# A rewritten first stage and an output stored by tile, in an mLSTM attention kernel with two dense layers

## The reference, cut to what is computed

```python
for t in range(S):
    m_new = np.maximum(f_gate[:, :, t] + m, i_gate[:, :, t])
    f_stab = np.exp(f_gate[:, :, t] + m - m_new)
    i_stab = np.exp(i_gate[:, :, t] - m_new)
    m = m_new
    C = f_stab * C + i_stab * outer(v_t, k_t)
    n = f_stab * n + i_stab * k_t
    y[:, :, t] = sigmoid(o_gate) * (C @ q_t) / maximum(abs(n @ q_t), 1.0)
h = x @ w_in                                   # 320 -> 2048
x = (maximum(h, 0) + alpha * minimum(h, 0)) @ w_out
out = maximum(maximum(x @ w1, x @ w2), x @ w3) @ w_out2   # 320 -> 768 -> 320
```

## Time and profile before

| | us |
|---|---|
| median of 3 runs | 790.53 (790.06 to 791.54) |
| the profiled execution | 790.44 |
| its span, first to last instruction | 788.7 |
| busy TensorE, VectorE, ScalarE, GpSimd | 742.5, 478.6, 309.9, 184.6 |

### The profile page before, as it was taken

How to read it: one execution, slowest core, us unless ns; L and a number is a source line. 1 busy time by engine, 2 the same in 40 slices (tenths; PEclk the granted TensorE clock), 3 DMA queues, 4 the chain that set the end, 5 groups by cost and what they waited for, 6 DMA issues and landing times.

```text
span 788.7 us, 11547 instructions
## 1 busy us (share of the span) xinstructions
PE 742.5 (94%) x4410; PEld 655.7 (83%) x4410; DVE 478.6 (61%) x823; ACT 309.9 (39%) x648; POOL 184.6 (23%) x187
## 2 busy tenths in 40 slices
PE   2556999999999999999999999999999999999997
PEld 2546999999998888888888888888888888888886
DVE  6456888878978786888688754934242332434222
ACT  4443465465456444644554245431111212121211
POOL 4376433335524332434233200000000000000000
PEclk9767999999999999999999999999999999999999
DMA  6961332222223221231110053030010202000000
GB/s 204 288 198 52 93 97 84 81 82 99 74 88 97 99 66 65 80 105 61 41 54 0 1 180 125 1 105 9 29 47 0 74 1 74 0 34 1 34 0 34
DMA packets 40057, 56.37 MB, mean 71 GB/s; under 512 B 3457, under 2 KB 29058, under 8 KB 39618
## 3 DMA queue, kind: packets, MB, share of 16 engines
q1 hardware_dynamic: 39570, 54.57, 22.0%
q10 hardware_dynamic: 432, 1.06, 0.4%
HBM read 47.65 MB, written 7.96 MB: 71 GB/s over the span
## 4 chain that ended last, share of the span: by engine, by line
PE 83%; DVE 7%; DMA 3%; POOL 3%; issue 1%; ACT 1%; SPq 1%; ACTq 0%; DVEq 0%; POOLq 0%
PE bank L664 25%; PE bank L628 20%; PE bank L642 5%; PE bank L643 5%; PE bank L644 5%; PE bank L554 4%; PE bank L678 3%; PE bank L679 3%; PE bank L680 3%; PE bank L646 3%; PE bank L647 3%; PE bank L562 1%; PE bank L569 1%; POOL wproj L369 1%; PE bank L591 1%
## 5 line engine op out<-in xcount | busy, mean ns | idle before, releaser
L628 PE MATMUL bank<-x_split,w_hi 128*128 128x512 f32 (+2 forms) x560 | 170.6, 372 | 2.2 <-ACT x_split L760 2.2
L628 PE MATMUL bank<-x_split,w_lo 128*128 128x512 f32 (+2 forms) x336 | 122.0, 365 | 0.0
L628 PEld LDWEIGHTS bank<-x_split,w_hi 128*128 128x128 f32 x560 | 103.8, 191 | 15.9 <-ACT x_split L760 2.6
L796 ACT ACTIVATE g_full<-bank 128x512 f32<-128x512 f32 (+2 forms) x112 | 59.7, 533 | 143.4 <-PE bank L628 141.7
L994 DVE SCALAR_TENSOR_TENSOR g_full<-g_full,beta,bank 128x512 f32<-128x512 f32 (+2 forms) x112 | 74.6, 667 | 38.2 <-ACT g_full L796 37.4
L642 PE MATMUL bank<-g_hi,wproj 128*128 128x512 f32 (+2 forms) x224 | 84.8, 379 | 4.0 <-DVE g_lo L975 4.0
L805 ACT ACTIVATE g_hi<-g_full 128x512 fp32r<-128x512 f32 (+2 forms) x112 | 63.1, 564 | 62.3 <-DVE g_full L994 62.1
L1015 DVE TENSOR_TENSOR best<-bank,first_of_max 128x512 f32<-128x512 f32 x36 | 24.9, 692 | 102.8 <-PE bank L664 76.4
L644 PE MATMUL bank<-g_hi,wproj 128*128 128x512 f32 (+2 forms) x224 | 81.3, 363 | 0.0
L643 PE MATMUL bank<-g_lo,wproj 128*128 128x512 f32 (+2 forms) x224 | 81.3, 363 | 0.0
L975 DVE TENSOR_TENSOR g_lo<-g_full,g_hi 128x512 fp32r<-128x512 f32 (+2 forms) x112 | 70.1, 626 | 18.1 <-ACT g_hi L805 17.3
(11 more groups left out here) (115 smaller groups left out, 1400.2 us busy)
## 6 DMA issues: line engine op xcount, KB each, us to landing
u_bcast<-u_scratch SPq DMA_DIRECT2D x24, 512.0 KB, 4.3
kv<-in_kv SPq DMA_DIRECT2D x24, 324.0 KB, 3.2
out<-final SPq DMA_DIRECT2D x6, 640.0 KB, 3.8
q_t<-in_q_t SPq DMA_DIRECT2D x24, 120.0 KB
k_t<-in_k_t SPq DMA_DIRECT2D x48, 60.0 KB
wproj_raw<-in_w_out SPq DMA_DIRECT2D x4, 640.0 KB, 9.6
o_gate<-in_o_gate SPq DMA_DIRECT2D x4, 640.0 KB, 5.0
w_raw<-in_w_max SPq DMA_DIRECT2D x2, 1152.0 KB, 6.5
```

The costliest lines, as they stand in the source:

```text
L628: ins = pe.matmul(ps[:, 0:cols], w[:, a, f], xs[:, x, 0:cols], start=(m == 0), stop=(m == 7))
L796: act.activation(gf[:, n % GF_SLOTS, 0:cols], hid[j % HID_BANKS][:, 0:cols], ACT.Relu, scale=-1.0).then_inc(neg_done, 1)
```

## The change

- **TensorE** starts with 20 products of zeros (`STILL`).
- **Gates** are worked out in two spans, chunks 0 and 1 of each batch, then chunks 2 to 5 (`SPANS`), in steps `chain`, `exps`, `turns` and `tables` that stand in the plan among the others.
- **u** of chunks 0 and 1 does not go through memory: TensorE spreads it by products with one-hot rows (`pick`) on top of a product that puts the mask there (`later`), and ScalarE reads it from PSUM. From chunk 2 on it is as before; ScalarE issues the store and the first load itself.
- **The decays** of the state come from a product with a one-hot row (`last`), in step `decays`, behind the first hidden tile of block 0; the state of chunk 1 is made after that (`late`). Chunk 0 needs no carry.
- **Weights** come in quarters, in the order in which block 0 uses them (`pieces`), all loaded by SP. All 16 low pieces are GpSimd's, each cut into operations of 256 columns (2 for one of w_in, 5 for one of w_out); the last eight lie around and inside block 0.
- **Loads**: chunk 1, the input gate and the first output gate are issued by ScalarE. Clearing of k moves from GpSimd to VectorE.
- **The end**: TensorE signals each of the last four tiles, ScalarE and VectorE copy two each, and each has its own store.

```diff
+ON_PE = PLAIN
+STILL = 20
+SPANS = [(0, ON_PE), (ON_PE, CPS)]
...
-    steps = [("prepare", 0), ("prepare", 1), ("gate", 0, 0), ("gate", 0, 1), ("scores", 0), ("carry", 0),
-             ("gate", 1, 0), ("gate", 1, 1), ("values", 0), ("scores", 1), ("finish", 0, 0), ("finish", 0, 1),
-             ("prepare", 2), ("carry", 1), ("values", 1), ("gate", 2, 0), ("gate", 2, 1), ("pack", 2, 0),
-             ("finish", 1, 0), ("finish", 1, 1), ("pack", 2, 1), ("prepare", 3)]
-    return steps + [("turn", 0), ("turn", 1)]
+    return [("chain", 0), ("exps", 0), ("turns", 0), ("bcast", 0), ("products", 0), ("tables", 0), ("gate", 0, 0),
+            ("gate", 0, 1), ("turns", 1), ("chain", 1), ("bcast", 1), ("scores", 0), ("tables", 1), ("prepare", 0),
+            ("chain", 2), ("values", 0), ("carry", 0), ("gate", 1, 0), ("gate", 1, 1), ("exps", 1), ("prepare", 1),
+            ("products", 1), ("scores", 1), ("finish", 0, 0), ("finish", 0, 1), ("carry", 1), ("values", 1),
+            ("turn", 0), ("turns", 2), ("finish", 1, 0), ("finish", 1, 1), ("tables", 2), ("turn", 1),
+            ("prepare", 2), ("gate", 2, 0), ("gate", 2, 1), ("pack", 2, 0), ("pack", 2, 1), ("prepare", 3)]
...
+        if b == 0 and n == 0:
+            both += [("decays",), ("late", 1)]
...
-PIECES = [("in", a, half) for half in range(2) for a in range(3)] + [("out", n, 0) for n in range(4)]
-ACT_PIECES = {("gate", 0, 1): (2, 3), ("gate", 1, 1): (3, 5), ("gate", 2, 1): (5, 6), ("pack", 2, 1): (6, 10)}
-DVE_PIECES = {("carry", 0): (2, 3)}
-POOL_PIECES = {("prepare", 2): (3, 5), ("prepare", 3): (5, 10)}
+    return [p for q in range(IN_PARTS) for p in [("in", a, q) for a in range(3)] + [("out", q, 0)]]
+ACT_PIECES = {("gate", 0, 1): (0, 3), ("exps", 1): (3, 7), ("turn", 0): (7, 8), ("gate", 2, 1): (8, 11),
+              ("hidden", 0, 1): (11, 12), ("hidden", 0, 2): (12, 15), ("hidden", 0, 3): (15, 16)}
+POOL_PIECES = {("prepare", 0): (0, 4), ("prepare", 1): (4, 8), ("pack", 2, 1): (8, 11), ("scores", 2): (11, 12),
+               ("carry", 2): (12, 15), ("carry", 3): (15, 16)}
+LOAD_U_AFTER = ("exps", 1)
...
+            sp.wait_ge(q_cleared, 1)
+            sp.wait_ge(k_cleared, 1)
+            load_chunk(sp, 0)
+            load_w1(sp, 0, range(3))
+            load_out(0)
+            load_w1(sp, 1, range(3))
+            sp.wait_ge(k_cleared, 3)
+            load_chunk(sp, 2)
+            load_out(1)
+            load_w1(sp, 2, range(3))
+            load_out(2)
+            load_w1(sp, 3, range(3))
+            load_out(3)
+            load_chunk(sp, 3)
+            sp.wait_ge(gates_done, 2)
+            for b in range(1, B):
+                store_u(sp, 0, b, u_stored[1])
+            sp.wait_ge(u_stored[0], 16)
+            load_u(sp, 3)
...
+            for n in range(STILL):
+                pe.matmul(ring[2][:, :], still[:, 0:128], still[:, :], start=True, stop=True)
...
+            def bcast(ch):
...
+                    for k in range(HG):
+                        pe.matmul(ps[:, k * L:(k + 1) * L], ident_b[:, :], later[:, :], start=(k == 0), stop=False,
+                                  skip_group_check=True)
+                    for k in range(HG):
+                        ins = pe.matmul(ps[:, k * L:(k + 1) * L], pick[:, g * HG + k, :], gates[:, U, t],
+                                        start=False, stop=True, skip_group_check=True)
...
             for s in PLAN_FIRST:
                 attention(s)
+                if s == LOAD_U_AFTER:
+                    act.wait_ge(u_stored[0], 16)
+                    load_u(act, ON_PE)
...
+            def last_tile(t):
+                act.wait_ge(tile2_out, t + 1)
+                act.activation(final[:, (NBLK2 - 1) % 2, t, :], acc2[t][:, 0:DM], ACT.Copy).then_inc(tile_ready[t], 1)
```

More of the change, by code:

```diff
@@ L222, in build @@
         end_at = cursor[0]
+        pick, _ = sb("pick_head", [128, H, L], F32, prob_r_at)
+        last, _ = sb("last_row", [128, 128], F32, prob_3_at)
+        later, _ = sb("later_keys", [128, 128], BF16, prob_3_at + 512)
+        ident_b, _ = sb("ident_bf16", [128, 128], BF16, prob_3_at + 768)
+        still, _ = sb("still", [128, 512], BF16, prob_at)
         cursor[0] = att_at
@@ L526, in drained, with decays @@
+            def decays():
+                pe.wait_ge(last_set, 1)
+                pe.wait_ge(tables_set, 3)
+                pe.matmul(acc[0][:, 256:256 + NCH * H], last[:, :], tables[:, 1, :, :].rearrange("p c h -> p (c h)"),
+                          start=True, stop=True).then_inc(decays_out, 1)
             def drained(n):
@@ L556, in attention @@
                         ins.then_inc(scored, 1)
-                if kind == "carry":
+                if kind == "carry" and ch:
                     ps = task("carry", ch)
@@ L564, in attention @@
                     ins.then_inc(carry_out, 1)
+                if (kind == "carry" and ch != 1) or kind == "late":
                     ps = task("state", ch)
@@ L673, in project2 @@
                 pe.wait_ge(g2_ready, b2 * J2 + f + 1)
+                last = b2 + 1 == NBLK2 and f + 1 == J2
                 for t in range(TT2):
@@ L720, in sigmoid, with exps @@
                 act.activation(og[:, b % 2, 0:n, :], og[:, b % 2, 0:n, :], ACT.Sigmoid).then_inc(o_done, 1)
-            sigmoid(0)
-            for half in range(2):
-                act.wait_ge(gates_done, half + 1)
-                if not half:
-                    ins = act.activation(gates[0:B * H, E, L:HALF], gates[0:B * H, U, L:HALF], ACT.Exp)
-                else:
-                    ins = act.activation(gates[0:B * H, E, HALF:S], gates[0:B * H, U, HALF:S], ACT.Exp)
-                for c in range(half * CPH, (half + 1) * CPH):
+            def exps(p):
+                first, end = SPANS[p]
+                act.wait_ge(gates_done, p + 1)
+                if p:
+                    store_u(act, ON_PE, 0, u_stored[0])
+                t = slice(max(first, 1) * L, end * L)
+                act.activation(gates[0:B * H, E, t], gates[0:B * H, U, t], ACT.Exp)
+                for c in range(first, end):
                     t = slice(c * L, (c + 1) * L)
@@ L733, in _ @@
                 ins.then_inc(exps_done, 1)
-                if not half:
-                    for n in range(2):
-                        high_piece(n)
+            sigmoid(0)
             def attention(step):
-                kind, ch = step[0], step[1]
+                kind = step[0]
+                if kind == "decays":
+                    return
+                ch = step[1]
                 c = ch % SLOTS
@@ L849, in _ @@
                 high2(b2, J2 - 1)
[L850 removed]
+                if b2 + 1 < NBLK2:
+                    final2(b2)
+            act.wait_ge(out_stored[(NBLK2 - 1) % 2], 16 * ((NBLK2 - 1) // 2))
+            for t in range(0, TT2, 2):
+                last_tile(t)
         @block.vector
@@ L895, in attention @@
             def attention(step):
-                kind, ch = step[0], step[1]
-                if kind in ("prepare", "gate", "pack", "sigmoid"):
+                kind = step[0]
+                if kind in ("prepare", "gate", "pack", "sigmoid", "exps", "turns", "bcast", "products"):
                     return
+                if kind == "decays":
+                    return set_decays()
+                ch = step[1]
+                if kind == "chain":
+                    return chain(ch)
+                if kind == "tables":
+                    return set_tables(ch)
                 c = ch % SLOTS
@@ L923, in attention @@
                                       .to_broadcast([128, NK, KH, DE]), ALU.mult).then_inc(carried_in, 1)
+                if (kind == "carry" and ch != 1) or kind == "late":
+                    if ch == 0:
+                        dve.wait_ge(own_set, 1)
                     ps = ring[TASKS.index(("state", ch)) % RING_BANKS]
```

402 lines of the change are left out of this document (240 added, 162 removed).

## The result

| | before | after |
|---|---|---|
| median, us | 791.03 (790.06 to 791.88, 4 runs) | 786.45 (785.84 to 787.38, 4 runs) |
| the profiled execution | 790.44 | 787.06 |
| its span | 788.7 | 785.1 |

The ratio is 0.9939, 95% interval 0.9923 to 0.9955: 4.6 us faster, where 9.5 were forecast. The profiled pair shows 3.4, because its run of before lies 0.6 under that median and its run of after 0.6 above. Single runs of one kernel differ by 1 to 2 us either way, so sums made from one profile can't be held to less than that.

The account below looks back on a forecast made before the run. TensorE was taken to set the pace from about 75 us on, so the front's shift counts: 790.44 - 9.7 (front) + 2.5 (back in block 0) - 2.2 (end) = 781.0 us, range 773.5 to 787.5.

Parts of the forecast that it names:

- What bounds the kernel: From about 75 us to the end only TensorE's own work sets the pace; a first-stage change shifts block 0's start.
- Gates and ScalarE up to the exponentials: First stage: first signal of the gates at 8.8, ScalarE's first gates from 11.6, exponentials of four chunks done at 20.5.
- The store of u: On ScalarE's own queue: leaves at 18.3, takes about 2.2 us, hidden up to 20.5.
- Rival (c): ScalarE's wait on u's store replaces the removed wait: at 7.23 us the chain starts 4.7 later, 785.7; chance 0.15.
- masks that wait for a DMA of u: Sign that the forecast is wrong: GpSimd's masks wait for this instead of for its own pieces.
- GpSimd as the chain of the front: GpSimd's 16 low pieces set the front: third state at 59.6 instead of 69.29, 9.7 us earlier.
- The zeros: 20 TensorE matmuls at the start speed chunk 0's broadcast: taken as 0, bounds a loss of 1.2 and a gain of 1.5.
- What comes back in block 0: GpSimd's pieces 12 to 15 inside block 0 contend with VectorE: 2.5 us back, bounds 0 and 7.9.
- The end: Last tiles' copies hidden behind TensorE, then a DMA of 160 KB: 2.2 us saved, 1.0 to 2.7.
- (b): GpSimd's quarter operations cost 0.59 instead of 0.72 and nothing comes back in block 0: 774.7; chance 0.2.
- (d): GpSimd and VectorE hold each other up in every small operation, 1.19 us each: 793.6, slower than before; chance 0.07.
- (e): u or weights land so late that block 0 starts where it did: 788.2, or 790.7 with 2.5 back; chance 0.03.

Follow-up runs that it names:

- the run with the weights held: SP holds the third quarter of w_in until u is stored, against the kernel with pieces put into the waits: 777.39 us, ratio 0.9833.
- the same kernel without the hold: After with low pieces 4 to 7 on VectorE, 8 to 10 moved ahead and 15 behind the pack of chunk 4: 777.47 us.
- with the wait moved: After with ScalarE's wait for the store of u and the load of u put behind high pieces 3 to 6: 782.21 us, ratio 0.9887.
- Filling the hole: After with 26 products of 256 columns added on TensorE ahead of the wait of project step 7 of block 0, for timing alone: 784.64 us.
- without any piece: After with the last four low pieces cut to 8 columns each, TensorE multiplying high parts in their place: 783.45 us, ratio 0.9910.
- piece 15 later: After with GpSimd's low piece 15 moved from behind the decay of chunk 3 to behind the last pack step of chunk 4: 785.58 us.
- VectorE's pieces: After with low pieces 4 to 7 moved from GpSimd to VectorE: 781.77 us; together with ScalarE's wait behind high pieces 3 to 6: 783.25 us.

## Why the prediction was half right

- **What bounds the kernel**: right. From rows to TensorE's last product nothing changed, 674.6 us in both.
- **Gates and ScalarE up to the exponentials**: right within 0.5 us (first products on gates at 8.96, forecast 8.8; first gate at 11.89, forecast 11.6; exponentials done at 21.0, forecast 20.5).
- **The store of u**: the step that failed. I gave it about 2.2 us of latency, hidden up to 20.5, because it has a queue to itself. It took from 18.88 to about 24.6, 5.7 us, and ScalarE stood still for 4.03. Rival (c) had this mechanism, at 4.7 later; the row of 7.23 us was there and should have been taken. That (c)'s 785.7 lies so near to 786.45 is in part luck: its wait is 0.7 too long (and counts the 0.4 for issuing the load on one side only), its block 0 gives back 2.4 too little. The sign that I gave for it, masks that wait for a DMA of u, did not show either; the wait sat on ScalarE, one step earlier. The store's own queue did not spare it the wait: DMA share in 20:30 was 1.09. The Trainium skill (DMA: Bandwidth & Descriptors, Queues, rings and completion order) says that each DMA engine takes its packets from the rows with work in turn. The trace agrees as far as the run with the weights held goes: 4.2 us from the issue of the store to that of the load behind it, against 5.9 in the same kernel without the hold. No run shows whether such turns make up the rest of the wait.
- **GpSimd as the chain of the front**: right in mechanism and size. From the late piece on my walk is off by 0.6 us in 36.6; a 256-column operation took 0.69 to 0.78 there, and with the wait moved the third state fell on 59.39.
- **The zeros**: taken as 0, measured at 2.1. The step said that ScalarE's list covers the broadcast until 11.6. At the slow rate it covers only the first half of it (ScalarE waits 1.10 us for the second), and not the scores behind it on TensorE, for which VectorE waits with the next gate chain behind it. My upper bound was 1.5. This adds nothing to the miss, since the forecast was for the kernel with the zeros.
- **What comes back in block 0**: 2.5 forecast, 4.9 measured, inside the bounds of 0 and 7.9. I had priced contention for VectorE's two-input operations and left out what follows. This is the second step that failed. One term was missing: VectorE operations that stand ahead of g_lo and are held up open a hole on TensorE (3.25 us), and behind it the clock is at half. Filling the hole gave 2.7 us of distance and 1.8 of the median. The last paragraph of my prediction named the clock as a sign but had no term for it.
- **The end**: right, 2.15 in the trace and 2.0 alone. Nothing between the last copy at 782.61 and the span's end at 785.1 but the issue and landing of 160 KB: 2.5 us, as taken.
- **Rivals (b), (d) and (e)**: GpSimd's 256-column operations cost neither 0.59 nor 1.19 but 0.69 to 0.78 on the chain, and 0.80 to 0.87 beside a busy VectorE. None of the three happened.

With the measured terms the sum closes, as it must, since they are all read from the two traces: 790.44 - 6.3 + 4.9 - 2.15 + 0.2 (1.96 us around the span instead of 1.74) = 787.1, the profiled run of after. Left open: the 1.8 to 2.0 us of distance that stay without any piece, and with piece 15 later (41.4 and 41.6 against 39.6). TensorE is idle 3.7 us on this way in both, against 1.7 before, so it is all idle time: without any piece nearly all in waits for g_lo, with piece 15 later 2.8 for g_lo and 0.8 for GpSimd's split. Part is a shift of my mark: GpSimd does piece 11 ahead of the decay, so at the third state g_lo is queued behind it on VectorE and TensorE stands for 0.4 to 0.9 us more, which it didn't before. The rest I did not separate.

The best kernels of the study take 777.4 to 777.5 us, 13.6 less than before and 9.0 less than after, with the same arithmetic and another order of the pieces.

## What to carry over

Before an engine that feeds a chain is made to wait for a DMA, count what stands behind the wait, and price the DMA by the slowest row under full queues, not by its size. Price a hole on TensorE by its length plus what the lower clock costs behind it (2.9 us behind one of 3.25 here, about 1.5 behind one of 3.22); a small VectorE operation ahead of TensorE's next operand can open one, so look at what GpSimd does beside it. When a chain is shortened, find the next arrival (here the broadcast of u at 33.5 to 34.3), and what will newly run side by side, before adding two gains.

## What the runs showed of the hardware

- From the issue of the 16 KB store of u on ScalarE's queue to the issue of the load that waits for it 5.7 us passed in after, where DMA share was 1.09 at 293 GB/s. In the other kernels that leave SP's loads alone it was 5.5 (the wait moved alone) to 7.2 (that and VectorE's pieces), with the weights held back 4.2. By the formula of the Trainium skill (DMA: Bandwidth & Descriptors, Anatomy of one DMA) the estimate is 2.0 us. The page fits it to single DMAs issued by GpSimd; this one is ScalarE's, under load, and the measurement decides.
- VectorE's operations on 128x8 values, 0.17 us alone, took 0.62 to 1.00 while GpSimd ran operations of 0.79 to 1.09 us beside them, in after and in the kernel without pieces. One of them (L1108) reads a single operand. An operation of 0.50 took 2.59 beside one of 2.38: in these rows VectorE's operation ends about when GpSimd's does. The kernel with the cut into 256 columns was 3.1 us faster, 2.1 of them behind the third state.
- It goes the other way too: GpSimd's mask of 1.11 us took 2.46 beside VectorE's pieces of 256 columns (0.36 each).
- After a hole of 3.25 us products of 256 columns took 0.41 us instead of 0.28, and the lower rate lasted from 84.04 to about 90.2; behind a hole of 3.22 us in another kernel it lasted from 80.40 to 83.7. What made the difference no run shows. 26 useless products in the hole kept the clock at 1.00.
- Without the zeros TensorE's first real work, from 9.0 us on, ran at about half the rate (eight products in 2.02 us instead of 1.11) and its first 16 score products, from 13.8 on, took 2.64 instead of 1.95, although the granted clock reads 1.00. The zeros lift a state that this column does not show.
